# Key products from high and low parts, two heads in turn, in a fused delta-rule attention and expert kernel

## The reference

```python
# 1. delta rule, token by token
k_n = k / (norm(k) + 1e-06)
for t in range(S):
    y[t] = q[t] @ state
    state = state + beta[t] * outer(k_n[t], v[t] - k_n[t] @ state)
# 2. a gated layer, 384 -> 2048 -> 384
h = x @ w_in;  x2 = (h * sigmoid(h)) @ w_out
# 3. one of 8 experts for each token with x2 @ w_skip > 0, 384 -> 1024 -> 384
out = x2;  out[chosen] = x2 + gate * (relu(x2 @ w1[e]) @ w2[e])
```

## Time and profile before

| | us |
|---|---|
| median of three runs | 973.23 |
| lowest, highest | 969.95, 973.46 |
| the profiled execution: its time | 974.0 |
| its span, from first to last instruction | 972.3 |
| PE busy, share of the span | 92% |
| DVE busy | 58% |
| ACT busy | 34% |
| POOL busy | 14% |
| mean granted TensorE clock | 0.963 of full speed |

### The profile page before, as it was taken

The page is one execution under the profiler, slowest core; times in us unless marked ns, Lnnn a source line. Parts: engine busy times, 40 slices in busy tenths (PEclk is TensorE's granted clock), DMA queues, the critical chain, the costliest instruction groups (busy, mean ns, idle before and its releaser), DMA issues.

```text
span 972.3 us, 25960 instructions
## 1 busy us (share of the span) xinstructions
PE 896.5 (92%) x10782; PEld 769.6 (79%) x10783; DVE 565.7 (58%) x1428; ACT 329.8 (34%) x779; POOL 140.3 (14%) x261
## 2 busy tenths in 40 slices
PE   4888999999999999999998999999999938999994
PEld 2466888888887788888887888888889927899894
DVE  4845765567645666477663766644442255677661
ACT  1531222323322233232322233232323335566551
POOL 3002000120001100021000210101000112354442
PEclk9798999999998999999999999999999968999997
DMA  7241110301221102211112111111004007566610
GB/s 253 85 133 39 40 61 13 106 23 51 78 78 39 42 33 78 77 52 45 56 40 78 56 39 56 56 33 42 18 18 147 18 33 266 173 187 222 203 39 12
DMA packets 36554, 75.71 MB, mean 78 GB/s; under 512 B 5530, under 2 KB 22376, under 8 KB 36448
## 3 DMA queue, kind: packets, MB, share of 16 engines
q1 hardware_dynamic: 33184, 69.53, 21.8%
q0 software_dynamic: 3264, 4.65, 1.5%
HBM read 63.50 MB, written 12.79 MB: 78 GB/s over the span
## 4 chain that ended last, share of the span: by engine, by line
PE 45%; issue 33%; POOL 8%; DMA 6%; DVE 4%; POOLq 2%; ACT 1%; SPq 0%
PE psum L702 5%; PE psum L820 5%; PE psum L796 5%; DMA kq_t<-x_table,ids_all 4%; PE psum L822 4%; PE psum L821 4%; PE psum L798 4%; PE psum L797 4%; POOL nrm L580 3%; PE psum L792 2%; PE psum L727 2%; PE psum L783 2%; PE psum L684 2%; DMA id_table<-token,slot 2%; PE psum L738 2%
## 5 line engine op out<-in xcount | busy, mean ns | idle before, releaser
L796 PE MATMUL psum<-xt_hi,w_hi 128*128 128x256 f32 x768 | 232.1, 302 | 7.5 <-issue 3.9
L949 ACT ACTIVATE h_raw<-psum 128x256 f32<-128x256 f32 x192 | 73.7, 384 | 443.8 <-PE psum L798 443.8
L797 PE MATMUL psum<-xt_lo,w_hi 128*128 128x256 f32 x768 | 217.4, 283 | 0.0
L798 PE MATMUL psum<-xt_hi,w_lo 128*128 128x256 f32 x768 | 217.1, 283 | 0.0
L1165 DVE TENSOR_TENSOR h_lo<-h_raw,h_hi 128x256 fp32r<-128x256 f32 x192 | 81.3, 423 | 200.3 <-ACT h_hi L950 199.6
L796 PEld LDWEIGHTS psum<-xt_hi,w_hi 128*128 128x128 f32 x768 | 145.8, 190 | 24.8 <-issue 18.2
L797 PEld LDWEIGHTS psum<-xt_lo,w_hi 128*128 128x128 f32 x768 | 146.5, 191 | 3.8 <-issue 3.8
L798 PEld LDWEIGHTS psum<-xt_hi,w_lo 128*128 128x128 f32 x768 | 146.6, 191 | 0.0
L820 PE MATMUL psum<-w_hi,h_hi 128*128 128x384 f32 x384 | 142.7, 372 | 0.2 <-DVE h_lo L1165 0.2
L822 PE MATMUL psum<-w_hi,h_lo 128*128 128x384 f32 x384 | 130.2, 339 | 0.0
L821 PE MATMUL psum<-w_lo,h_hi 128*128 128x384 f32 x384 | 129.8, 338 | 0.0
(11 more groups left out here) (169 smaller groups left out, 1305.0 us busy)
## 6 DMA issues: line engine op xcount, KB each, us to landing
kq_t<-kq SPq DMA_DIRECT2D x24, 512.0 KB, 4.2
bp<-moe_w SPq DMA_DIRECT2D x24, 512.0 KB, 4.2
kv_t<-kv SPq DMA_DIRECT2D x24, 384.0 KB, 3.2
bp<-moe_w SPq DMA_DIRECT2D x24, 384.0 KB, 4.5
kd<-kq SPq DMA_DIRECT2D x22, 256.0 KB, 3.7
x_table<-x_sb SPq DMA_DIRECT2D x12, 392.0 KB, 2.5
out<-x_sb SPq DMA_DIRECT2D x12, 384.0 KB, 2.4
bp<-moe_w_in SPq DMA_DIRECT2D x6, 512.0 KB, 6.8
```

The costliest lines, as they stand in the source:

```text
L796: m(out, hi, x_hi, start=first, stop=False)
L797: m(out, hi, x_lo, start=False, stop=False)
L798: return m(out, lo, x_hi, start=False, stop=last)
L949: a_.activation(h_raw[i % 2][:, :], up_ps[i % 2][:, 0:G2], ACT.Silu)
```

## The change

`gram` takes two heads in a call. The key and query tile is split into `kq_hi` (rounded to float32r, by ScalarE) and `kq_lo` (what is left, by VectorE), and a head's product is the sum of three float32r matmuls: high by high, high by low, low by high. The two heads' matmuls alternate. `parts` stands in slot j = 11, for the step after next. `bp` has two buffers in place of three; the space is that of the two new tiles. The weights' stage is one `bp` buffer and two of the three key tiles. In SyncE's order the keys of step 0 come ahead of the weights, behind a wait for the second key tile, and those of step 1 behind the last weights. The root is taken on VectorE by a bit shift and three Newton steps, 12 small operations more. The order of the work is dealt anew, for quad 0 in another way than for the rest.

```diff
-        bp = [sb(f"bp{i}", [P, H, 2, C]) for i in range(NB)]
+        NBP = 2
+        bp = [sb(f"bp{i}", [P, H, 2, C]) for i in range(NBP)]
+        kq_hi = sb("kq_hi", [P, 2, HP, C], F32R)
+        kq_lo = sb("kq_lo", [P, 2, HP, C], F32R)
...
-        stage = bp_half[2:6]
+        stage = bp_half[2:4] + [kq_t[i][:, :, :, :].rearrange("p s h c -> p (s h c)") for i in (1, 2)]
...
-        def gram_ps(h):
-            return psum[:, 4 + h % 2, 0:2 * C].rearrange("p (s c) -> p s c", s=2)
+        def gram_ps(t, h):
+            return psum[:, 4 + h % (4 if t == 0 else 2), 0:2 * C].rearrange("p (s c) -> p s c", s=2)
...
-        LANE_SLOTS = range(17, 58)
-        GRAM_AT = {6: 0, 7: 2, 8: 4, 10: 6}
+        LANE_SLOTS = range(30, 58), range(22, 58)
+        PREPARE = ({18: [("squares", (0,))], 20: [("squares", (1,))], 24: [("norms", (0,))], 25: [("norms", (1,))],
+                    27: [("turn", ())], 28: [("norms", (2,))], 29: [("spread", ())]},
+                   {9: [("squares", (0,))], 11: [("squares", (1,))], 13: [("turn", ())], 14: [("norms", (0,))],
+                    15: [("norms", (1,))], 17: [("norms", (2,))], 21: [("spread", ())]})
+        GRAM_AT = {6: 0, 7: 1, 8: 2, 10: 3}
+        PARTS_AT = 11
...  the prelude
+            s["parts"](0)
             for n in range(2):
                 s["weights"](n)
             s["turn"](0)
-            s["norms"](0)
+            for n in range(3):
+                s["norms"](0, n)
+            for hp in range(2):
+                s["gram"](0, hp)
+            for n in range(2, 4):
+                s["weights"](n)
             s["spread"](0)
             s["scales"](0)
-            for h in range(H):
-                s["gram"](0, h)
+            for hp in range(2, HP):
+                s["gram"](0, hp)
             for k in range(1, Q - 1):
                 s["lanes"](0, k)
-                if k % 2 and 2 + k // 2 < WP:
-                    s["weights"](2 + k // 2)
+                if k % 2 and 4 + k // 2 < WP:
+                    s["weights"](4 + k // 2)
+            s["warm"](24, WP - 1)
             s["turn_back"](0)
+            s["parts"](1)
...  the slots
-                    if t + 1 < T and j == 13:
+                    if t + 1 < T and j == 12:
                         s["scales"](t + 1)
-                    if p == 0:
-                        s["warm"](6)
+                    if t + 2 < T and j == PARTS_AT:
+                        s["parts"](t + 2)
+                    if p == 0 and j < 12:
+                        s["warm"](6, WP)
...  SyncE
             def load_kq(t):
                 after(sp, pu_done, t - NB + 1)
+                if t in (1, 2):
+                    sp.wait_ge(w_rest, WP)
...
             sp.dma_start(beta_t[:, :], beta).then_inc(beta_in, 16)
+            sp.wait_ge(kd_in[1], 16)
+            load_kq(0)
             for i in range(2):
                 load_weights(i)
             load_kv(0)
-            load_kq(0)
...
-            load_kq(1)
             for i in range(NSTAGE, WP):
                 load_weights(i)
+            load_kq(1)
             load_kd(4)
...  TensorE
-                after(pe, bp_ready, H * t + h - 1)
...
-                m(gram_ps(h), kq_t[i][rows, 0, h // 2, :], kq_t[i][rows, :, h // 2, :],
-                  start=True, stop=True).then_inc(gram_done, 1)
+                if hp == 0:
+                    pe.wait_ge(kq_lo_ready, t + 1)
...
+                after(pe, bp_ready, H * t + 2 * hp - (0 if t else 2))
+                for n, (left, right) in enumerate(((kq_hi, kq_hi), (kq_hi, kq_lo), (kq_lo, kq_hi))):
+                    for a in range(2):
+                        rows = slice(DP * a, DP * a + DP)
+                        last = m(gram_ps(t, 2 * hp + a), left[rows, 0, hp, :], right[rows, :, hp, :], start=n == 0, stop=n == 2)
+                        if n == 2:
+                            last.then_inc(gram_done, 1)
...  ScalarE
+            def parts(t):
+                act.wait_ge(kq_in[t % NB], 16 * (t // NB + 1))
+                after(act, gram_done, H * t)
+                cp(kq_hi[:, :, :, :], kq_t[t % NB][:, :, :, :]).then_inc(kq_hi_ready, 1)
...  VectorE
+                bits = root[:, :].bitcast(I32)
+                if part == 0:
+                    then(d.tensor_scalar(bits, nsq[:, :].bitcast(I32), 1, None, ALU.logical_shift_right))
+                    then(d.tensor_scalar(bits, bits, -1.0, float(0x5f3759df), ALU.mult, ALU.add))
+                for three in ((3.0,), (12.0, 768.0), ())[part]:
+                    then(d.tensor_tensor(rinv[:, :], nsq[:, :], root[:, :], ALU.mult))
+                    then(d.tensor_tensor(rinv[:, :], rinv[:, :], root[:, :], ALU.mult))
+                    then(d.scalar_tensor_tensor(root[:, :], rinv[:, :], -three, root[:, :], ALU.add, ALU.mult))
+                if part == 1:
+                    then(d.tensor_tensor(root[:, :], root[:, :], nsq[:, :], ALU.mult))
...
+            def parts(t):
+                dve.wait_ge(kq_hi_ready, t + 1)
+                d.tensor_tensor(kq_lo[:, :, :, :], kq_t[t % NB][:, :, :, :], f32(kq_hi[:, :, :, :]), ALU.subtract).then_inc(kq_lo_ready, 1)
```

More of the change, by code:

```diff
@@ L82, in program @@
         nsq = sb("nsq", [P, LN])
-        nrm = sb("nrm", [P, LN])
+        root = sb("root", [P, LN])
         rinv = sb("rinv", [P, LN])
@@ L284, in lane_count, with lane_slots @@
             return (2 * (Q - 2)) * g + 2 * (k - 1)
[L288 to L289 removed]
+        LANE_SLOTS = range(30, 58), range(22, 58)
[5 more added lines that the diff above has]
+        PARTS_AT = 11
         def spare(x):
             x, j = x % SLOTS, x % (SLOTS // 2)
[L293 removed]
+            used = 4 * (x % 2 == 0) + 6 * (j in (0, 2, 4, 6, 10)) + 8 * (j == 8) + 9 * (j in GRAM_AT) + 11 * (j == 12) + 12 * (j == PARTS_AT) + 16 * (x == 16) + 13 * (x == 19)
             return max(1, 18 - used)
[L296 removed]
+        def lane_slots(slots):
             cost = [2 * (k * (Q - 1 - k) + 151) for k in range(1, Q - 1)]
[L299 to L300 removed]
+            share = sum(cost) / sum(spare(x) for x in slots)
+            run, x, room, where = 0, slots[0], spare(slots[0]) * share, {}
             for k, c in enumerate(cost, 1):
[L302 removed]
+                while run + c / 2 > room and x < slots[-1]:
                     x += 1
@@ L307, in lane_slots @@
             return where
-        LANES = lane_slots()
+        LANES = [lane_slots(slots) for slots in LANE_SLOTS]
         CHAIN = {0: ("read", 0), 1: ("solve", 0), 2: ("carry", 1), 3: ("solve", 1), 4: ("carry", 2), 5: ("solve", 2),
@@ L359, in schedule @@
                                 s["evict"](g + 1, a)
-                        if z in (9, 10):
-                            s["squares"](g + 1, z - 9)
-                        if z == 12:
-                            s["turn"](g + 1)
-                        if z == 14:
-                            s["norms"](g + 1)
-                        if z == 15:
-                            s["spread"](g + 1)
-                        for k in LANES.get(z, ()):
+                        for name, n in PREPARE[g > 0].get(z, ()):
+                            s[name](g + 1, *n)
+                        for k in LANES[g > 0].get(z, ()):
                             s["lanes"](g + 1, k)
@@ L410, in steps @@
             names = [name for name, _ in CHAIN.values()]
-            names += ["diag", "evict", "squares", "norms", "spread", "scales", "gram", "turn", "lanes", "turn_back", "weights", "up", "lo", "down",
+            names += ["parts", "diag", "evict", "squares", "norms", "spread", "scales", "gram", "turn", "lanes", "turn_back", "weights", "up", "lo", "down",
                       "x2", "x2t", "logits", "choose", "rank", "place", "first", "warm"]
@@ L598, in place @@
                                          oob_is_err=False).then_inc(id_stored, 16)
-            schedule(steps(squares=squares, turn=turn, place=place))
+            schedule(steps(turn=turn, place=place))
             hold(id_stored, 32 * NP)
@@ L973, in first @@
                 split(0, 0, x)
-            schedule(steps(spread=spread, solve=solve, keep=keep, weights=weights, up=up, x2=x2, x2t=x2t,
+            schedule(steps(spread=spread, parts=parts, solve=solve, keep=keep, weights=weights, up=up, x2=x2, x2t=x2t,
                            first=first))
@@ L1058, in squares, with norms @@
                     d.tensor_reduce(nsq[:, :], inv[:, :, :], AX.X, ALU.add).then_inc(sq_done, 1)
-            NORM = 5
-            def norms(g):
-                n = [NORM * g]
+            NORM = 17
+            NORM_PART = (0, 5, 12)
+            def norms(g, part):
+                n = [NORM * g + NORM_PART[part]]
                 def then(ins):
@@ L1232, in first @@
                 split(0, x, 0)
-            schedule(steps(evict=evict, squares=squares, norms=norms, scales=scales, spread=spread, gram=gram, turn=turn, lanes=lanes, turn_back=turn_back, read=read, carry=rest,
```

(1 more changed line is left out.)

81 lines of the change are left out of this document (37 added, 44 removed).

## The result

The changed kernel takes 981.96 us (median of 7 runs, 978.03 to 986.77) where the kernel before takes 973.23 (7 runs, 969.58 to 974.66): a ratio of 1.01, interval 1.0072 to 1.0127. It is 1% slower; 956 was forecast. The profiled execution took 980.42, its span is 978.7.

The account below looks back on a forecast made before the run. PE's stream was taken to bound the gated layer's pairs, VectorE chains the prelude and pair 0. -14.5 + 4.8 + 1 - 6 - 1.5 - 7 + 6 = -17.2 from 974.0 gives 957, 956 as a median; range 943 to 967.

Parts of the forecast that it names:

- Part 1: Products in pairs 1 to 11: `gram` call falls from 0.63 to 0.35 to 0.45; 63 calls by 0.23, 14.5 us saved.
- one call in four: The `gram` call at j = 8, which waits 0.26 for VectorE's `bp`; 63 of 84 calls were counted as saving.
- Part 2: VectorE's and ScalarE's added work: 4.8 us lost at quad hand-overs in pairs 2, 4, 6, 8, and 1 for denser lanes.
- hidden on average: VectorE's 3.8 us more per pair, on 34 to 40 busy of 57, was taken as hidden on average.
- at nothing: ScalarE's added 1.06 us operation per step: no cost, as only slot 12's `up` copies stand behind, over a slot to spare.
- the hand-over at slot 16 to 17: Pairs 2, 4, 6, 8: PE's wait for `rest`, 0.64 before, grows; 1.2 us more lost each, 4.8 in all.
- My signs of being wrong: Call above 0.55, no idle stretch ahead of step 2's solve, or `rest` waits over 10 us in pairs 1 to 11.
- Rival (a): Pairs 1 to 11: VectorE becomes the bound, each of 21 steps loses 0.5, 10 us more, 966; chance 0.15.
- Rival (d): Products gain nothing, as the call's hand-overs cost what the columns save, 0.6 a call, 970; chance 0.05.
- (b): `gram` calls: the two heads don't overlap in float32r, 63 calls lose 0.18 each, 982; chance 0.06.
- (c): Pair 0's backlog isn't there and the first stop goes: 6 + 2.5 us more saved, 947; chance 0.15.
- Parts 3 and 4: Prelude: 6 us saved to solve, 1.5 at the first stop. Pair 0: 7 saved, then 6 lost ahead of step 2.

Follow-up runs that it names:

- e2: Changed kernel with `turn_back` in slot 61 of a quad in place of 59: 974.22 us, ratio 0.999 to the kernel before.
- e11: e2 with GpSimd's power for the root and pair 0's work for quad 1 dealt to two places: 959.5 us, 0.9836 of the kernel before.
- e6: e1 plus one VectorE operation over 128x1024 in slot 11 of each step, its result unread: 976.01 us, 1.0021 of the kernel before.
- e3: Changed kernel with one head's three matmuls ahead of the other's, not alternating: 985.19 us, 1.0101 of the kernel before.
- e8: e1 with quad 1's preparation dealt to slots 6 to 9 of step 0 and 19 to 23 of step 1: 958.31 us, 0.9847 of the kernel before.
- e12: Changed kernel with VectorE's low part at the end of slot 11, behind its other work there: 978.0 us, 0.9985 of the kernel before.
- e1: Changed kernel with float32 products and no split, the rest of the change kept: 966.02 us, 0.9892 of the kernel before.

## Why the prediction was wrong

**Part 1, a term mis-sized.** I read 0.63 as "two and two with a 0.1 hand-over, or only the middle two at once", and took a hand-over of 0 to 0.1 for the new call. The hand-overs are 0.1 on both sides after, and by the sum above before too, so that the heads overlapped fully already. The steady part goes from 0.43 to 0.35, and with it 0.08 a call; at 0.55 the call stands on the bound above which I had called the prediction wrong. I also took one call in four to give nothing back, because of the 0.26 at j = 8. That was misread: before and after, 0.27 lies between the last `down` matmul and every call behind it, 0.09 more than between two `down` matmuls, and no wait for `bp` grew. At every j a call without a stop in it went from 0.63 or 0.64 to 0.54 to 0.56. 84 calls by 0.08 are 6.7 us in place of 14.5.

**Part 2, the step that failed.** The forecast lost 5.8 here. The waits for VectorE grew by 16.5. Two things in it were wrong. First, I wrote that VectorE's additions are "hidden on average" and checked one follower, `rest` of slot 16. `h_lo` of the gated layer comes every slot, and it is the follower of what stands in slot 59; I passed over "turn back + parts" there, and e2 shows that this one clump is worth 1.1%. Second, ScalarE's part was costed "at nothing" because ScalarE has slots to spare. ScalarE had, but VectorE stands next to it in the same slot and waits:

```profile
DVE kq_lo L1133 <- ACT kq_hi L914: 9.9, 19, 0.5
```

19 times 0.5 us, with all of VectorE's work queued behind (the waits of VectorE after, 130 to 745). One thing was right: the hand-over at slot 16 to 17, 0.64 before, became 1.6, 0.95 more and near the 1.2 of the forecast, from the queue that I had listed (e11 shows that it takes the split and the Newton steps together). My own working there, 0.6 to 0.9 and 0.7 more, gives 1.3 to 1.6 and not 1.2.

My signs of being wrong missed it too: the call is not above 0.55, the idle stretch is there, and the waits for `rest` are 8.9, under 10. I had set a sign for the one follower that I had checked.

**Rival (a) is nearest to what happened.** Its 10 us beside the 5.8 of part 2 are 15.8 of waits, and 16.5 more were measured; that these lie so close is luck, for I had it evenly over the steps, 0.5 in each, and it stands in nine places. It gave 966 only because part 1's 14.5 still stood in its sum. I held 30 to 40% of free time against it. In 618 us VectorE is busy 396, 64%, and TensorE still waits 1.6 to 1.8 us for it nine times: its free time lies where it waits for `h_hi` (134 us of it), not where the clumps are. e6 shows it without the split. Rival (d) was nearly right on the call. (b) gave the right total, 982, by luck: e3 and the call's own starts refute its mechanism. (c) is refuted by the 8.87.

**Parts 3 and 4 held.** The lanes start at 28.45 (forecast 29.7), solve of step 0 at 52.50 (54.1), the first stop shrank from 5.65 to 2.75, step 1 gained 7.6 (7), and step 2 gave back 7.5 (6), with 8.87 of idle where 7 to 8 were forecast; the solve behind it takes 0.54 in place of 0.37, at a granted clock of 0.78 from 95 to 105. What I did not see is that this backlog could be dealt to two places (e8), worth 10 us by the end of step 2 in the traces (114.96 against 125.33), though less in the whole.

**The sum of pairs 1 to 11:** 16.5 of waits, less 6.7 for the calls, less 0.9 in stops without a releaser, is 8.9 of the 12.4 measured. The other 3.5 can be estimated, and were not tested. A wait is listed from the end of the matmul ahead, and that end lies 0.16 behind the point where the next one would have started: at 276.82 above a matmul starts, the next would follow 0.12 later, and it starts at 278.94, a loss of 2.00 where 1.84 is listed. After has 11 waits more than before, 1.8 us in all. And the granted clock reads 0.97 in four stretches of 60 us after, where before has 0.94 in one and 0.97 in another: some 1.8 us more. Both are small beside what one trace can be trusted for (small stops alone moved by 2.5 between e12 and after).

**The bounds.** The upper saving was added wrongly: 84 calls at 0.28 are 23.5, 9 more than 14.5, and with part 2 at nothing that is 14.8 better and not 12 to 13. It does not bear on the miss, which lies on the other side: for the losses I allowed twice 5.8, and the waits were nearly three times that.

## What to carry to other kernels

Price an added operation by what stands behind it on its in-order engine in that slot, at its worst slot, not by the engine's mean share of free time; and list what each edit drops into the same slot, since two harmless moves there (a new operation and a 2 us transpose) cost more than the gain. A pass saved is worth only its columns: split the group that it is in into steady part and hand-overs before multiplying. Where a change has several parts, run each alone, and then in pairs: here the order of the first 130 us was worth 6 us with e1 and 16 with e8 (by the end of step 2, in the traces), and the split that the change is named for cost 2% more than it gave beside the Newton steps and the transpose, but some half a percent without them.

## What was not expected of the hardware

- The order of the matmuls of two 64-row halves makes no difference to their overlap: 0.55 a call alternating and one head after the other.
- A group of 64-row matmuls between 128-row ones costs about 0.1 us at its start and again at its end (0.22 and 0.21 for passes that take 0.12), and as much in its neighbours: the next start comes 0.27 after that of the last `down` matmul ahead, where it is 0.17 between two of them, and 0.22 after that of the first `up` matmul behind, where it is else 0.12. The neighbours' part is the same before and after. The Trainium skill says in "TensorEngine Tiling (Array Packing)", section "Key Properties", that changing the tiling mode drains the engine; the trace agrees and gives the price.
- A GpSimd tensor-tensor operation over 128x1024 took 2.34 to 2.81 us (VectorE: 1.22), and two groups of VectorE's two-input operations on SBUF went from 423 to 500 ns and from 551 to 937 ns on average, by a few that lasted as long as GpSimd's, while `rest`, with one input in PSUM, stayed at 0.55. The Trainium skill names this contention in "GPSIMD Engine Reference", section "1. Specifications": the ports are shared with VectorE's instructions that have two SBUF inputs. The trace agrees.
